# Attention, MLP and gated convolution on one core: the phases of the first MLP cut from batches to half batches

## The reference

```python
scores = scale * q @ k.T            # per head, scale 1/8
mask   = (rel >= 0) & (rel < 128)   # rel = query - key; window of 128
scores = where(mask, scores - slope[h] * rel, -1e9)
x      = softmax(scores) @ v        # heads side by side: 512 features

xn     = (x - mean) / sqrt(var + 1e-6) * g_ln
x      = x + relu(xn @ w_ch1) @ w_ch2          # 512 -> 2048 -> 512

h      = relu(x @ w_in)                        # 512 -> 1024
gate   = sigmoid(3-tap convolution of h along the tokens)
out    = (h * gate) @ w_out                    # 1024 -> 512
```

## Time and profile before

| | us |
|---|---|
| median of 3 runs | 839.34 |
| lowest, highest | 838.4, 842.31 |
| the profiled execution | 845.15 |
| its span, first to last instruction | 843.4 |

### The profile page before, as it was taken

One profiled execution on the slowest core, in us unless ns is written; L12 is line 12 of the kernel. 1 busy time (PEld: TensorE's weight loads), 2 busy tenths in 40 slices (PEclk: granted clock), 3 DMA queues, 4 the chain that ended last, 5 costly groups with the idle time before them and its releaser, 6 DMA issues.

```text
span 843.4 us, 17148 instructions
## 1 busy us (share of the span) xinstructions
PE 812.5 (96%) x5871; PEld 770.4 (91%) x5871; DVE 521.1 (62%) x1420; ACT 371.9 (44%) x1031; POOL 177.3 (21%) x170
## 2 busy tenths in 40 slices
PE   9999877999989999998999999999999999999998
PEld 5668776999979999998999999999998999999998
DVE  2556665777447777745677764422228977788862
ACT  4626543566323556522466541222325544444442
POOL 5437772122012112101022110011110110111100
PEclk9999999999989999999999999999999999999999
DMA  5415432222031222112212301411212022221201
GB/s 145 121 45 155 129 85 85 71 74 67 3 120 38 63 72 72 37 58 67 65 50 57 100 9 57 136 57 41 88 52 85 22 79 84 77 77 35 70 23 43
DMA packets 56111, 59.30 MB, mean 70 GB/s; under 512 B 24800, under 2 KB 43232, under 8 KB 55520
## 3 DMA queue, kind: packets, MB, share of 16 engines
q1 hardware_dynamic: 56032, 58.30, 23.4%
HBM read 44.12 MB, written 14.16 MB: 69 GB/s over the span
## 4 chain that ended last, share of the span: by engine, by line
PE 80%; issue 9%; DVE 7%; ACT 2%; POOL 1%; ACTq 0%; DVEq 0%; POOLq 0%
PE bank L1303 22%; PE bank L1305 20%; PE bank L1304 20%; PE bank L1274 3%; PE bank L1242 3%; PE bank L1256 3%; PE bank L1203 2%; PE bank L1194 2%; PE bank L1227 2%; PE bank L1216 1%; PE bank L1286 1%; DVE q_st L1054 1%; PE bank L1295 1%; ACT prob L744 1%; DVE prob L966 1%
## 5 line engine op out<-in xcount | busy, mean ns | idle before, releaser
L1303 PE MATMUL bank<-xn_hi,wa_hi 128*128 128x288 f32 x512 | 158.1, 309 | 3.4 <-issue 1.9
L1303 PE MATMUL bank<-h_hi,wb_hi 128*128 128x288 f32 x512 | 158.3, 309 | 0.5 <-DVE ch_stage L1034 0.5
L1304 PE MATMUL bank<-xn_lo,wa_hi 128*128 128x288 f32 x512 | 152.7, 298 | 0.0
L1305 PE MATMUL bank<-xn_hi,wa_lo 128*128 128x288 f32 x512 | 152.4, 298 | 0.0
L1304 PE MATMUL bank<-h_lo,wb_hi 128*128 128x288 f32 x512 | 151.7, 296 | 0.0
L1305 PE MATMUL bank<-h_hi,wb_lo 128*128 128x288 f32 x512 | 151.5, 296 | 0.0
L1023 DVE SCALAR_TENSOR_TENSOR h_lo<-bank,h_hi 128x288 fp32r<-128x288 f32 x128 | 58.3, 455 | 120.2 <-ACT h_hi L774 118.8
L774 ACT ACTIVATE h_hi<-bank 128x288 fp32r<-128x288 f32 x128 | 52.5, 410 | 176.2 <-PE bank L1305 175.3
L1303 PEld LDWEIGHTS bank<-xn_hi,wa_hi 128*128 128x128 f32 x512 | 97.6, 191 | 7.3 <-issue 5.0
L1303 PEld LDWEIGHTS bank<-h_hi,wb_hi 128*128 128x128 f32 x512 | 97.2, 190 | 4.5 <-issue 2.9
L1304 PEld LDWEIGHTS bank<-xn_lo,wa_hi 128*128 128x128 f32 x512 | 97.8, 191 | 0.0
(11 more groups left out here) (127 smaller groups left out, 1721.3 us busy)
## 6 DMA issues: line engine op xcount, KB each, us to landing
w_stage<-w SPq DMA_DIRECT2D x32, 256.0 KB, 2.9
k_raw<-qkT SPq DMA_DIRECT2D x48, 144.0 KB, 2.9
q_raw<-qkT SPq DMA_DIRECT2D x48, 144.0 KB, 2.9
x_in<-x_spill SPq DMA_DIRECT2D x8, 580.0 KB, 4.4
ch_in<-ch_spill SPq DMA_DIRECT2D x8, 580.0 KB, 5.3
x_spill<-xT SPq DMA_DIRECT2D x4, 1152.0 KB, 4.2
ch_spill<-ch_stage SPq DMA_DIRECT2D x32, 144.0 KB, 2.1
out<-out_stage SPq DMA_DIRECT2D x32, 144.0 KB, 1.8
```

Source lines behind the costliest of these rows:

```text
L1303: nc.tensor.matmul(dst, w_h, a_h, start=start, stop=False)
L1304: nc.tensor.matmul(dst, w_h, a_l, start=False, stop=False)
L1305: last = nc.tensor.matmul(dst, w_l, a_h, start=False, stop=stop)
```

## The change

Every phase now covers one chunk of the first MLP, 32 slots, with the attention and the norm of the next chunk beside it. `prologue`: chunk c0 of batch 0, still in plain fp32, with ten weight tiles and three instead of four fillers in six places. `first`: MLP of batch 0's c0 beside the attention of its c1, now in the split form, and 22 weight tiles, of which VectorE makes every fourth low part. A hardware loop of three passes holds `one` (MLP c1 of batch b, attention c0 of batch b + 1) and `zero` (MLP c0 and attention c1 of batch b + 1). `last`: MLP of batch 3's c1 with the sixteen tiles of the second MLP's weights and the first two loads of its input.

A half head has its own tiles and parts: c0 three score tiles of 128, 256 and 192 keys and outputs of 256, 192 and 64 columns; c1 two tiles of 256 keys and outputs of 256, 128 and 128 columns. No padding is left. The transposed probabilities fill one bank and take one copy and one subtraction. The probabilities have three buffers, q, k and v raw data two, q and k come in one transfer of 128 partitions (doubled in the input array on the host), and the ch spill of a chunk is one transfer. Heads start every 2.6 slots, the norm of the chunk at slot 24.2.

```diff
+TILES = ([(128, 0, 128, 128, 0), (128, 0, 256, 0, 128), (64, 128, 192, 0, 384)],
+         [(128, 0, 256, 0, 0), (128, 128, 256, 0, 256)])
...
+GROUPS = ([[(0, 0), (1, 128)], [(2, 0)]], [[(0, 0), (1, 256)]])
...
+BLOCKS = ([(0, 0, 0), (1, 0, 128), (1, 128, 256), (2, 0, 384), (2, 128, 448)],
+          [(0, 0, 0), (0, 128, 128), (1, 0, 256), (1, 128, 384)])
+
+PARTS = ([(0, 128, 0, 256, 0), (1, 128, 256, 192, 128), (2, 64, 448, 64, 256)],
+         [(1, 128, 128, 256, 0), (0, 128, 0, 128, 0), (2, 128, 384, 128, 128)])
...
+HEAD0, HEAD_SLOT = 0.9, 2.6
+AT = {("S", 0): 0.0, ("S", 1): 1.1, ("PT", 0): 2.95, ("O", 0): 4.35}
+D_NORM = (1.8, 1.4)
+PREP_AT, PREPV_AT = 1.5, 2.0
+NORM_AT = 24.2
+NORM_TIMES = {("IN", 0): 0.0, ("IN", 1): 1.0, ("OUT", 0): 2.8, ("IN", 2): 3.3, ("OUT", 1): 4.2, ("OUT", 2): 5.2}
+SPILL_X_AT = 24.6
...
+WARM = [(1.79, 8)] + [(m + 0.78, 3) for m in range(2, H)] + [(H + 0.3, 4), (H + 0.7, 3), (H + 1.2, 4), (H + 1.7, 6)]
+WARM += [(NORM_AT_PROLOGUE + t, n) for t, n in ((0.3, 9), (0.6, 4), (0.9, 4), (1.2, 4))]
...
+W_PROLOGUE = 10
+FIRST_W, W_SLOT, W_PACE = 0.9, 0.95, 1.1
...
+    return n < W_PROLOGUE or (n % 4 != 3 if n < NW1 else n % 2 == 1)
...
+MLP_C = {"first": 0, "one": 1, "zero": 0, "last": 1}
+ATT_C = {"prologue": 0, "first": 1, "one": 0, "zero": 1}
...
+        out = head_items(0, 0.0, 1.0, AT_PROLOGUE) + norm_items(NORM_AT_PROLOGUE, NORM_TIMES_PROLOGUE)
+        out += [(FIRST_W + W_SLOT * n, ("W", n)) for n in range(W_PROLOGUE)] + [(t, ("WARM", n)) for t, n in WARM]
+        return sorted(out, key=lambda y: y[0])
...
+    if kind != "last":
+        c = ATT_C[kind]
+        out += head_items(c, HEAD0, HEAD_SLOT, AT) + norm_items(NORM_AT, NORM_TIMES)
+        out += [(HEAD0 + HEAD_SLOT * (h - 1) + PREP_AT if h else -0.95, ("PREP", h)) for h in range(H)]
+        out += [(HEAD0 + HEAD_SLOT * (h - 1) + PREPV_AT if h else -0.9, ("PREPV", h)) for h in range(H)]
     if kind == "first":
...
-        halves = half_items(1, HALF0, HALF_SLOTS, HALF_FIRST, range(H))
-        out += [(t, x) for t, x in halves if x[0] != "HS" or x[2] >= EARLY_HALVES]
-        out += norm_items(FIRST_NORM_0, 1, NORM_TIMES_0) + head_items(FIRST_HEAD_0, HEAD_SLOTS_0) + norm_items(LAST_NORM_0, 0)
-        out += [(X_SPILL_AT, ("X",)), (LOAD_AT, ("LOAD",))]
-    elif kind == "steady":
-        out += norm_items(FIRST_NORM, 1) + head_items(FIRST_HEAD, HEAD_SLOTS) + norm_items(LAST_NORM, 0)
-    else:
-        out += norm_items(FIRST_NORM, 1)
-        out += [(2 * (F1 + m) + 1, ("W", NW1 + m)) for m in range(NW2)]
-        out += [(12.2, ("Y", 0)), (22.2, ("Y", 1))]
-    return sorted(out, key=lambda x: x[0])
+    if kind in ("first", "zero"):
+        out += [(SPILL_X_AT, ("X",))]
+    if kind in ("one", "zero", "last"):
+        out += [(1.0, ("C",))]
+    if kind == "last":
+        out += [(2 * m + 1.0, ("W", NW1 + m)) for m in range(NW2)]
+        out += [(6.2, ("Y", 0)), (16.2, ("Y", 1))]
+    return sorted(out, key=lambda y: y[0])
...
+        def phases(run, eng):
+
+            run("prologue", None, 0)
+            run("first", 0, 0)
+            with eng.Fori(0, B - 1) as b:
+                run("one", b, b + 1)
+                run("zero", b + 1, b + 1)
+            run("last", B - 1, None)
...
+                sp.dma_start(qk_raw[:, h % 2, :, 0:KEYS[c]], qkT[b, h, :, :, KEY0[c]:KEY0[c] + KEYS[c]]).then_inc(qk_loaded[h % 2], 16)
...
+                sp.dma_start(ch_dram[b, :, :, CH * c:CH * (c + 1)], ch_stage[:]).then_inc(ch_spilled, 16)
...
+                nc.scalar.activation(pt_hi[:], bank_of(b, c, ("PT", h, 0))[:], ACT.Copy).then_inc(pt_hi_ready, 1)
...
+            def scores(b, c, h, x):
+                dst = take_bank(b, c, ("S", h, x))
+                if x == 0:
+                    pe.wait_ge(q_split, head_no(b, c, h) + 1)
+                    pe.wait_ge(k_split, head_no(b, c, h) + 1)
+                for t, at in GROUPS[c][x]:
+                    rows, k0, keys, _, _ = TILES[c][t]
+                    for part in (k_hi, k_lo):
+                        last = nc.tensor.matmul(dst[0:rows, at:at + keys], q_st[:, P * t:P * t + rows],
+                                                part[:, k0:k0 + keys], start=part is k_hi, stop=part is k_lo)
...
-                    rows, k0, keys, _ = TILES[t]
-                    keys = max(keys, 192)
-                    for part in (k_hi, k_lo):
-                        last = nc.tensor.matmul(dst[0:rows, 256 * i:256 * i + keys], q_st[:, P * t:P * t + rows],
-                                                part[:, k0:k0 + keys], start=part is k_hi, stop=part is k_lo)
-                last.then_inc(bank_filled, 1)
...
-                    parts = [(0, PT0, 256, 0), (1, PT1, 256, 128), (2, PTZA + 64, 192, 192)]
-                else:
-                    parts = [(2, PT2 + 128, 192, 0), (3, PT3, 192, 0), (4, PTZB, 192, 0)]
-                for i, (j, src, cols, col) in enumerate(parts):
+            def outputs(b, c, h):
+                dst = take_bank(b, c, ("O", h, 0))
+                pe.wait_ge(v_split, head_no(b, c, h) + 1)
+                pe.wait_ge(pt_ready, head_no(b, c, h) + 1)
+                for i, (j, n, src, cols, col) in enumerate(PARTS[c]):
                     for pt in (pt_hi, pt_lo):
-                        last = nc.tensor.matmul(dst[:, col:col + cols], v_st[:, j, :], pt[:, src:src + cols],
+                        last = nc.tensor.matmul(dst[:, col:col + cols], v_st[0:n, h % 2, j, :], pt[0:n, src:src + cols],
                                                 start=i == 0 and pt is pt_hi, stop=i == 2 and pt is pt_lo,
                                                 skip_group_check=True)
                 last.then_inc(bank_filled, 1)
...
-            warm(WARM_START, bank[7])
-            run("prologue", 0)
-            run("first", 0)
-            with pe.Fori(0, B - 2) as b:
-                run("steady", b + 1)
-            run("last", B - 1)
...
+            phases(run, pe)
```

More of the change, by code:

```diff
@@ L36 @@
 LN_TILES = CH // LT
[L37 to L55 removed]
+LEAD = 1
+SMALL, GAP = 41, 240
 NSTAGE = 4
@@ L102 @@
-WARM += [(H + 2.3 + t, n) for t, n in ((0.3, 9), (0.6, 4), (0.9, 4), (1.2, 4))]
-D_APPLY = {"prologue": 0.22, "first": 1.3, "steady": 1.1, "last": 1.1}
-X_SPILL_AT, LOAD_AT = 22.0, 5.0
-W_PROLOGUE = 8
-FIRST_W, W_SLOTS, W_PACE = 0.9, 1.15, 0.85
-LEAD_GAIN_PROLOGUE = 0.5
-assert W_PROLOGUE % 2 == 0
-def head_items(start, slots=6.0, frame=FRAME, lag=LAG):
-    out = []
-    for n in range(H + max(lag.values())):
-        for (kind, x), at in frame.items():
-            h = n - lag[kind]
-            if 0 <= h < H:
-                out.append((start + slots * (n + at / 6), (kind, h, x)))
-    return out
@@ L148, in mlp_groups, with norm_items @@
+def norm_items(start, times):
+    return [(start + t, (kind, j)) for (kind, j), t in times.items()]
 def mlp_groups():
@@ new lines, with phase_of, use_base @@
+assert USES["first"] == USES["zero"]
+N_USES = {k: len(v) for k, v in USES.items()}
+PAIR = N_USES["one"] + N_USES["zero"]
+assert N_USES["first"] % 2 == 0 and N_USES["one"] % 2 == 0
+def phase_of(b, c):
+    if isinstance(b, int) and b == 0:
+        return ("first" if c else "prologue"), 0
+    return ("zero", b) if c else ("one", b - 1)
+def use_base(kind, bm):
+    if kind == "prologue":
+        return 0
+    if kind == "first":
+        return N_USES["prologue"]
+    first = N_USES["prologue"] + N_USES["first"]
+    return first + PAIR * bm if kind == "one" else first + PAIR * (bm - 1) + N_USES["one"]
@@ L558, in _ @@
+            phases(run, sp)
             last = B - 1
@@ L837, in _ @@
                 nc.scalar.activation(out_stage[:, i, 1:2], ident[:, 0:1], ACT.Copy).then_inc(out_staged, 1)
-            run("prologue", 0)
-            half_normalise(1, 0)
-            run("first", 0)
-            with act.Fori(0, B - 2) as b:
-                run("steady", b + 1)
-            run("last", B - 1)
+            phases(run, act)
             def relu2(n, c, f, first=False):
@@ L1102, in _ @@
             nc.vector.memset(out_stage[:, 1, 2:3], 0.0).then_inc(ch_dve, 1)
-            run("prologue", 0)
-            half_inverse(1, 0)
-            run("first", 0)
-            with dve.Fori(0, B - 2) as b:
-                run("steady", b + 1)
-            run("last", B - 1)
+            phases(run, dve)
             def convolve(n, c, f):
```

1166 lines of the change are left out of this document (478 added, 688 removed).

## The result

The changed kernel takes **894.4 us** (median of 4 runs, 892.4 to 900.9) beside 840.1 for the kernel before on the same chip: ratio 1.066, 95% interval 1.059 to 1.072. It is slower; I had forecast 816, with 0.73 for faster.

The account below looks back on a forecast made before the run. TensorE was taken as the bound. Stage, attention, loop-edge and wait terms summed to 820.4 us, 23.0 less than the profiled span of 843.4; the same difference from the 839.34 median gave 816 us, range 803 to 838.

Parts of the forecast that it names:

- Waits in the other phases: TensorE's extra waits in the six phases outside "first": 1 us more per phase, 6 us, ends 0 and 30.
- VectorE's order takes over: Rival: in c0 half heads VectorE's chain between scores and transposes overruns its slots, TensorE waits: 845 us, chance 0.14.
- Waits in "first": TensorE's waits left in the new phase "first": 6 us, from 2 to 20.
- Loads of the last phase: Weight tiles from the fifth on stand behind a load of x: should cost nothing, at most 2 us.
- Prologue: Stage before the MLP, with fewer fillers and no early chunk 1 scores: 56.9 us instead of 59.49.
- the narrow matmuls: Rival: attention's 128- and 64-column matmuls run at the plain fp32 rate: +27 us, 838 in all, chance 0.15.
- The back edges: The loop's back edge is taken twice instead of once, TensorE idle 1.52 us each: 3.0 us in the sum.
- The second MLP: Stage after the last phase, not touched by the change: 211.4 us.
- the half heads themselves: Attention of batches 1 to 3: same TensorE cost as before, 4.12 us per head, 98.9 us in all.

Follow-up runs that it names:

- e3_lastloads: Changed kernel with the second MLP's weight tiles 36 to 39 loaded ahead of the x load that waits for the first y: 887.9 us.
- e5_unroll: Changed kernel with the loop over the pairs of half batches written out on all engines, no order changed: 890.6 us.

## Why the prediction was wrong

- **Waits in the other phases: the step that failed.** "I take 1 us more per phase for six, 6 us." It measured 10.4 us in each "one" and 3.8 in each "zero" (84.3 and 73.7, against 73.9 and 69.9 once the order is mended): 43 us, some 3 for the edges and perhaps 4 for the tile height among them. That is the rival "VectorE's order takes over", which I priced at 845 with 0.14: its place was right (the low part of the next q ahead of the scaling, the transposes waiting), its size and its reach were not, for the heads of chunk 1 wait too. I set 4.3 us of chain against 4.7 of slot; in the head shown above the chain took 5.6, and TensorE's own work only 4.2. The scalings with their sums I had right (1.5; from 362.37 to 363.86 it is 1.49). I left out the sum of the previous output, whose bank the transposes need (0.54 with its handover), and counted the low part of an MLP block (0.47) only as a remark; q's low part took 0.91 instead of 0.75, and the minimum began 0.50 after the scores instead of 0.25. And I argued against it from the fewer instructions per head and from TensorE's small idle time in the old loop. Neither says anything of the order: the transposes come 1.85 slots behind the last scores now, where the old loop left 2.6 or more. The end of 30 us that I gave the term was not far enough either.
- **Waits in "first".** I took 6, from 2 to 20. 15 more than that sum came, so the end of the range was just passed. I looked at GpSimd's load (5.0 of 5.8 us) and held that it "fits"; it does, but beside GpSimd's work VectorE's takes longer, which I had not priced.
- **Loads of the last phase.** "It should cost nothing, at most 2 us": 6.3, and all of it back in e3_lastloads.
- **Prologue.** 56.9, measured 60.75, and 52.7 to 57.2 once the scaling comes first. The faster pace of the weight tiles moved one past a scaling on GpSimd's queue, and that I had not followed.
- **Right:** the narrow matmuls. Outputs of a chunk 1 head in the changed kernel (TensorE's timeline):

```profile
415.73 0.22 PE L1047 MATMUL bank<-pt_hi,v_st 128*128 128x128 f32 x1
415.79 0.27 PE L1047 MATMUL bank<-pt_lo,v_st 128*128 128x128 f32 x1
415.90 0.28 PE L1047 MATMUL bank<-pt_hi,v_st 128*128 128x128 f32 x1
416.01 0.27 PE L1047 MATMUL bank<-pt_lo,v_st 128*128 128x128 f32 x1
```

  With 128 columns the second starts 0.06 us after the first, and the others follow at 0.11 (I took 0.108), so that rival falls; only the change to a tile of 64 rows, some 0.26 us per chunk 0 head, was missing. The back edges: 3.0, measured 1.62 and 1.24, and 3 back in e5_unroll. The second MLP 211.4, measured 211.05. And, nearly, the half heads themselves: with the order mended the passes come within 6 us of the sum, 4.6 us a pair.

## What to carry to other kernels

When a schedule gives two dependent steps fewer slots, list everything that stands between them on each in-order engine, the previous and the next item's work included, and the readers of the bank that the later step takes; set its sum against the slots, and where it "fits by little", price it as a wait in every round. Include the waits of one engine for another: VectorE stood idle inside the chain. Fewer instructions per head, or an engine that is busy for 60% of the time, is no argument. And a schedule that lost may still be sound: here the change with its due times, loads and loop set anew went from 6.6% slower to about 1% faster than the kernel before.
